# Second MLP: first and second products' matmuls alternate one by one, and the first products' two PSUM banks change places each step

## The chip, the cores and the metric

One core of one Trainium2 chip runs the whole program. The metric is the device time of one execution in microseconds; the median of three executions of the kernel before is 850.15 us (850.1 to 851.2).

## What is computed

The reference runs windowed attention over 4 batches of 8 heads with 576 positions of 64 values, and passes the result, as 2304 tokens of 512 values, through two MLPs with a hidden width of 2048:

```python
def _moe_ref(x, w_in, w_out):            # first MLP
    h = np.maximum(x @ w_in, 0.0)
    return (h * h @ w_out).astype(np.float32)

def _moe2_ref(x, w_in, w_out):           # second MLP
    h = x @ w_in
    g = h * np.cos(h)
    return (g @ w_out).astype(np.float32)
```

## The kernel before

Attention takes the first 100 us or so. Both MLPs work in steps: a block of 768 tokens has 8 steps, each for 256 hidden columns. Step numbers n run from 0 to 47; `FRESH` = 24 is the first of the second MLP, `second(n)` says whether n is in it, and j = n % 8 is the place in the block.

**First products** (x times w_in, `hidden_product(n, i)`, line 706). A 2 by 2 block product is made with seven products, not eight. Each is six matmuls of 384 columns: two halves of the contraction, and for each hi*hi, hi*lo and lo*hi of values split in a rounded and a rest part. Product i writes PSUM bank i % 2. Products 0, 1 and 4 start a fresh sum, the others add on top of what lies in their bank, so each bank has to be read out at the right moment: ScalarE copies the result of product 0 to `part_a` (`copy_part`, line 882, semaphore `part_a_ready`) and that of product 2 to `hidden_sum` (`copy_first_sum`, line 886); VectorE adds in `part_b_sum`, `part_c_sum`, `c22_sum`, `c21_sum` and `c12_sum` (lines 1286 to 1301, in this order `sum_done` goes up by five a step) after products 1, 3, 4, 5, 6. The waits of TensorE stand in lines 723 to 734: product 0 for all five sums of the step before, product 2 for `part_a`, 3 for part_b_sum, 4 for copy_first_sum, 5 for part_c_sum, 6 for c22_sum.

**Between the products.** The hidden values of a step lie in four quarters i of 384 columns. In the second MLP each passes h * cos(h) by nine instructions of the two engines: ScalarE `turns` and `whole` (number of full turns, line 937), VectorE `turn_high` and `turn_low` (take them off, line 1307), ScalarE `absolute` and `cosine` (line 955), VectorE `make_g` (times h, line 1320), ScalarE `round_g` (rounded part, line 965), VectorE `lo_g` (rest part, line 1335). Quarter 0 comes from copy_first_sum, 1 from c22_sum, 2 from c21_sum, 3 from c12_sum.

**Second products** (g times w_out, `second_product(q)`, line 756). Two for each step, each of six pieces of three matmuls with 512 columns in the second MLP. It is a Python generator that gives one piece at a time. `mlp_step(n)` (line 803) runs the seven first products and puts pieces behind them as `pieces_after` says: the six pieces of product 2n-4 (`old`) and then the six of 2n-1 (`new`). Inside the second MLP, but for j = 1 and 2, that is six pieces after product 2 and six after product 6: two rows. `new` needs quarters 1 and 2 of step n-1.

**What sets the order.** Each engine runs its own instruction list, written out by hand; `second_step(n)` has one for ScalarE (line 1027) and one for VectorE (line 1468). Semaphores with constant counts join the lists. SyncE starts all loads in its own order. Beside the quarters, both lists carry `round_moving`, `moving_sum` and `split_moving`, which prepare the next block's operands.

Of the kernel before, what the change touches and what calls it, by code (L numbers as in the profile page):

```python
# [6 lines left out]

# [2 lines left out]

# [6 lines left out]
ALU = mybir.AluOpType  # L19
# [99 lines left out]
def attention_mlp_kernel(nc, q_t, k_t, v, w_in1, w_out1, w_in2, w_out2, out):  # L119
    with ExitStack() as ctx:  # L120
# [170 lines left out]
        def second(n):  # L291

            return n >= ALL // 2

        def slab(q):

# [270 lines left out]
        def _(pe):  # L567
# [135 lines left out]
                last = product(1, 8, keys_at(1, 3 * P + HALF, upper), TAIL_AT[1] + HALF, final=True)  # L703
                last.then_inc(pv_done, 1)

            def hidden_product(n, i):

                t, r = n // STEPS, n % 2
                weight, moving = PRODUCTS[i].split("*")
                w, m = COMB.index(weight), moving  # L710
                if n < MADE:
                    if i < 2:
                        pe.wait_ge(comb_ready, 2 * n + i + 1)
                elif i in GROUP_FIRST:
                    pe.wait_ge(comb_landed[r][GROUP_FIRST[i]], 16 * ((n - MADE) // 2 + 1))
                if n == 0:
                    if m in FIRST_LO_POOL:
                        pe.wait_ge(first_lo_ready, FIRST_LO_POOL[m])
                    if m in FIRST_LO_DVE:
                        pe.wait_ge(xt_ready, FIRST_LO_DVE.index(m) + 1)  # L720
                elif n % STEPS == 0:
                    pe.wait_ge(xt_ready, lo_done(t, m))
                if i == 0 and n > 0:
                    pe.wait_ge(sum_done, 5 * n)
                elif i == 2:
                    pe.wait_ge(part_a_ready, n + 1)
                elif i == 3:
                    pe.wait_ge(sum_done, 5 * n + 1)
                elif i == 4:
                    pe.wait_ge(first_sum_ready, n + 1)  # L730
                elif i == 5:
                    pe.wait_ge(sum_done, 5 * n + 2)
                elif i == 6:
                    pe.wait_ge(sum_done, 5 * n + 3)
                first = i in (0, 1, 4)
                for k in range(2):
                    cols = slice(k * P, k * P + P)
                    hi, lo = comb[:, r, 0, w, cols], comb[:, r, 1, w, cols]
                    for wi, mi in ((hi, moving_hi(t, m)), (hi, moving_lo(t, m)), (lo, moving_hi(t, m))):
                        last = pe.matmul(psum[:, H_BANK + i % 2, 0:NH], wi, mi[:, k, :], start=first, stop=True,  # L740
                                         skip_group_check=True)
                        first = False
                last.then_inc(product_done, 1)

            def wait_for_bank(t, c):

# [9 lines left out]
            def second_product(q):  # L756

                n, r = q // 2, q % W_RING
                t, start = n // STEPS, q % (2 * STEPS) == 1
                final = q == FINAL  # L760
                wo, wl = wout[:, r, 0, :], wout[:, r, 1, :]
                for c in range(6 if second(n) else 4):
                    if c == 0:
                        if second(n):
                            pe.wait_ge(wout_landed[r], 16 * (q // W_RING + 1))
                        else:
                            pe.wait_ge(wout_ready, y_order(q))
                        pe.wait_ge(g_ready, 4 * n + (3 if q % 2 else 4))
                    if start and t > 0:
                        wait_for_bank(t, c)  # L770
                    if second(n):
                        tok = slice(c * P, c * P + P)
                        for m, (g, w) in enumerate(((g_hi, wo), (g_hi, wl), (g_lo, wo))):
                            last = pe.matmul(psum[:, Y_BANK + c, :], g[:, r, tok], w, start=start and m == 0, stop=True,  # L774
                                             skip_group_check=True)
                    else:
                        w = slice(c * P, c * P + P)
                        for m, (wi, g) in enumerate(((wo, g_hi), (wo, g_lo), (wl, g_hi))):
                            pe.matmul(psum[:, Y_BANK + c, :], wi[:, w], g[:, r, 0:512], start=start and m == 0, stop=True,  # L779
                                      skip_group_check=True)  # L780
                            last = pe.matmul(psum[:, Y_BANK + 4 + c // 2, 256 * (c % 2):256 * (c % 2) + 256], wi[:, w],  # L781
                                             g[:, r, 512:N], start=start and m == 0 and c % 2 == 0, stop=True,
                                             skip_group_check=True)
                    if c == (5 if second(n) else 3):
                        last.then_inc(second_done, 1)
                    elif final:
                        last.then_inc(y_done, 1)
                    yield

            def pieces_after(n, i):  # L790

                old, new = second(n - 2), second(n - 1)
                if n <= 2:
                    return ((0, 1, 1, 1, 1, 0, 1), (1, 1, 0, 0, 1, 1, 2))[n - 1][i]
                if n % STEPS == 1:
                    if i < 2:
                        return 3 if old else 2
                    return ((0, 0, 2, 2, 2) if new else (0, 1, 1, 1, 1))[i - 2]
                if old:
                    return ((2, 1, 2, 1, 2, 2, 2) if n % STEPS == 2 else (0, 0, 6, 0, 0, 0, 6))[i]  # L800
                return (1, 1, 1, 1, 1, 1, 2)[i]

            def mlp_step(n):
                old = second_product(2 * n - 4) if n > 2 else zeroth
                new = second_product(2 * n - 1) if n > 1 else first
                olds = 2 if n % STEPS == 1 and n > 1 else 4
                for i in range(len(PRODUCTS)):
                    hidden_product(n, i)
                    for _ in range(pieces_after(n, i)):
                        if n == 1:  # L810
                            next(new if i < 4 else old)
                        else:
                            next(old if i < olds else new)

            zeroth, first = second_product(0), second_product(1)

# [24 lines left out]
            values(PAIRS - 1)  # L841
            hidden_product(0, 6)
            pe.wait_ge(x_ready, PAIRS)
            next(first)
            for n in range(1, ALL):
                mlp_step(n)
            for q in (2 * ALL - 4, 2 * ALL - 1, FINAL):
# [4 lines left out]
        def _(act):  # L852
# [28 lines left out]

            def copy_part(n):
                act.wait_ge(product_done, 7 * n + 1)
                act.activation(part_a[:], psum[:, H_BANK, 0:NH], ACT.Copy).then_inc(part_a_ready, 1)  # L884

            def copy_first_sum(n):

                act.wait_ge(product_done, 7 * n + 3)
                if n > 0:
                    act.wait_ge(g_done, 4 * (n - 1) + 1)  # L890
                act.activation(hidden_sum[:, 0, :], psum[:, H_BANK, 0:NH], ACT.Copy).then_inc(first_sum_ready, 1)

            def weights_hi(n):
                r = n % 2
# [132 lines left out]
            def second_step(n):  # L1027
                t, j = divmod(n, STEPS)
                if n == FRESH:
                    copy_part(n)  # L1030
                    round_g(n - 1, 2)
                    round_wout(2 * n - 2)
                    round_g(n - 1, 3)
                else:
                    whole(n - 1, 3)
                    if n < ALL:
                        copy_part(n)
                    round_g(n - 1, 1)
                    absolute(n - 1, 2)
                    cosine(n - 1, 2)  # L1040
                    round_g(n - 1, 2)
# [70 lines left out]
        def _(dve):  # L1112
# [166 lines left out]
                dve.tensor_tensor(wout[:, r, 1, :], wout_raw[:, r, 1, :], wout[:, r, 0, :].bitcast(F32), ALU.subtract)\  # L1279
                    .then_inc(wout_ready, 1)  # L1280

            def sum_of(n, product, bank, left, to):
                dve.wait_ge(product_done, 7 * n + product + 1)
                dve.tensor_tensor(to, psum[:, H_BANK + bank, 0:NH], left, ALU.add).then_inc(sum_done, 1)  # L1284

            def part_b_sum(n):
                dve.wait_ge(part_a_ready, n + 1)
                sum_of(n, 1, 1, part_a[:], part_b[:])

            def part_c_sum(n):  # L1290
                sum_of(n, 3, 1, part_a[:], part_c[:])

            def c22_sum(n):
                dve.wait_ge(sum_done, 5 * n + 2)
                sum_of(n, 4, 0, part_c[:], hidden_sum[:, 1, :])

            def c21_sum(n):
                sum_of(n, 5, 1, part_a[:], hidden_sum[:, 2, :])

            def c12_sum(n):  # L1300
                sum_of(n, 6, 0, part_b[:], hidden_sum[:, 3, :])

            def quarter(n, i):

# [163 lines left out]
            def second_step(n):  # L1468
                t, j = divmod(n, STEPS)
                if n == FRESH:  # L1470
# [2 lines left out]
                    split_wout(2 * n - 2)  # L1473
                    lo_g(n - 1, 3)
                    split_at(n)
                else:
                    make_g(n - 1, 1)
                    turn_low(n - 1, 2)
                    lo_g(n - 1, 1)
                    turn_high(n - 1, 3)  # L1480
# [97 lines left out]
```

## Time and profile before

| | us |
|---|---|
| median of three executions | 850.15 |
| the profiled execution | 850.42 |
| its span | 848.3 |
| TensorE busy in the span | 836.8 |
| VectorE busy | 647.5 |
| ScalarE busy | 520.3 |
| one step (step 39) | 15.60 |

The span is from the first to the last instruction of the profiled execution. A busy share is an average over all stages; the second MLP runs from about 458 us to the end. Step 39 starts at 691.9 us.

### The profile page before, as it was taken

To read this page: it belongs to the slowest core of one execution; us is meant where nothing else is said; L and a number is where in the kernel's file an instruction comes from. 1 tells how busy PE (TensorE), PEld (TensorE's weight loads), DVE (VectorE), ACT (ScalarE), POOL (GpSimd) and SP (SyncE) were. 2 spreads that over 40 slices of the span, in tenths; PEclk is the share of its full clock that TensorE was granted. 3 is DMA by queue.
4 is the path that set the end of the run, shared out by engine and by line. 5 is a ranking of instruction groups with operands and counts; after the bars stand their busy time and mean duration, and the time that the engine had idled before them with its cause. 6 is when DMAs were issued, how large, how long until landed. Compare 5 with 4: busy or idle time off the path is not lost.

```text
span 848.3 us, 16158 instructions
## 1 busy us (share of the span) xinstructions
PE 836.8 (99%) x5846; PEld 759.9 (90%) x5846; DVE 647.5 (76%) x1448; ACT 520.3 (61%) x1148; POOL 84.4 (10%) x177
## 2 busy tenths in 40 slices
PE   8999999999999999999999999999999999999998
PEld 6777999999999999999999999899889989899996
DVE  7999888886696775786766787777787677677665
ACT  7999454432343333344333887877787777787775
POOL 7999400000000000000000000000000000000000
PEclk9999999999999999999999999999999999999999
DMA  7776736457679779769868556555575655675522
GB/s 245 253 255 183 254 117 245 173 170 276 226 271 321 254 244 322 275 238 317 288 242 295 182 198 200 182 171 194 189 254 181 200 183 175 211 241 177 191 75 75
DMA packets 72190, 185.34 MB, mean 218 GB/s; under 512 B 7216, under 2 KB 19760, under 8 KB 70064
## 3 DMA queue, kind: packets, MB, share of 16 engines
q1 hardware_dynamic: 71248, 183.23, 64.2%
q10 hardware_dynamic: 864, 1.08, 0.4%
q8 instruction: 47, 0.77, 0.4%
q14 instruction: 31, 0.25, 0.1%
HBM read 141.82 MB, written 42.47 MB: 217 GB/s over the span
## 4 chain that ended last, share of the span: by engine, by line
PE 89%; DVE 7%; POOL 2%; issue 1%; ACT 1%; DVEq 0%; POOLq 0%
PE psum L740 40%; PE psum L774 23%; PE psum L779 15%; PE psum L781 8%; DVE probs L1152 3%; POOL probs L528 2%; DVE pt L1172 1%; DVE guarded L1161 1%; PE psum L632 1%; PE psum L679 1%; PE psum L574 1%; DVE x L1180 0%; ACT probs L861 0%; DVE x L1179 0%; PE psum L591 0%
## 5 line engine op out<-in xcount | busy, mean ns | idle before, releaser
L740 PE MATMUL psum<-xt_hi,comb 128*128 128x384 f32 x1344 | 381.3, 336 | 0.2
L740 PEld LDWEIGHTS psum<-xt_hi,comb 128*128 128x128 f32 x1344 | 246.4, 188 | 10.7 <-DVE hidden_sum L1284 0.4
L774 PE MATMUL psum<-wout,g_hi 128*128 128x512 f32 x576 | 178.4, 391 | 0.0
L1338 DVE TENSOR_TENSOR g_lo<-work,g_hi 128x384 fp32r<-128x384 f32 x192 | 102.4, 552 | 74.1 <-ACT g_hi L971 72.7
L779 PE MATMUL psum<-g_hi,wout 128*128 128x512 f32 x384 | 148.8, 391 | 0.0
L971 ACT ACTIVATE g_hi<-work 128x384 fp32r<-128x384 f32 x192 | 97.6, 519 | 70.1 <-DVE work L1333 42.2
L740 PE MATMUL psum<-x_lo,comb 128*128 128x384 f32 x384 | 128.6, 335 | 0.0
L774 PEld LDWEIGHTS psum<-wout,g_hi 128*128 128x128 f32 x576 | 107.2, 188 | 19.0
L774 PE MATMUL psum<-wout,g_lo 128*128 128x512 f32 x288 | 113.2, 393 | 0.0
L781 PE MATMUL psum<-g_hi,wout 128*128 128x256 f32 x384 | 107.5, 280 | 0.0
L884 ACT ACTIVATE part_a<-psum 128x384 f32<-128x384 f32 x48 | 23.6, 491 | 125.5 <-PE psum L740 125.5
L740 PE MATMUL psum<-xt_lo,comb 128*128 128x384 f32 x288 | 96.6, 335 | 0.0
L779 PEld LDWEIGHTS psum<-g_hi,wout 128*128 128x128 f32 x384 | 71.9, 187 | 9.0
L779 PE MATMUL psum<-g_lo,wout 128*128 128x512 f32 x192 | 75.1, 391 | 0.0
L740 PEld LDWEIGHTS psum<-x_lo,comb 128*128 128x128 f32 x384 | 72.2, 188 | 1.6
L947 ACT ACTIVATE angle<-hidden_sum,consts 128x384 f32<-128x384 f32 x96 | 58.4, 609 | 22.8 <-DVE hidden_sum L1284 21.9
L781 PEld LDWEIGHTS psum<-g_hi,wout 128*128 128x128 f32 x384 | 72.4, 188 | 0.0
L528 POOL TENSOR_SCALAR probs<-probs,inverse 128x128 f32<-128x128 f32 (+1 forms) x144 | 68.7, 498 | 9.6 <-DVE inverse L1164 9.6
L861 ACT ACTIVATE probs<-probs,neg_max 128x128 f32<-128x128 f32 (+1 forms) x144 | 61.9, 438 | 4.2 <-DVE neg_max L1152 4.2
L774 PEld LDWEIGHTS psum<-wout,g_lo 128*128 128x128 f32 x288 | 54.0, 188 | 11.4
L1311 DVE SCALAR_TENSOR_TENSOR work<-angle,hidden_sum 128x384 f32<-128x384 f32 x96 | 52.9, 551 | 13.9 <-ACT angle L953 13.9
L1284 DVE TENSOR_TENSOR part_b<-psum,part_a 128x384 f32<-128x384 f32 x48 | 26.6, 554 | 48.3 <-PE psum L740 48.3
(99 smaller groups left out, 1267.6 us busy)
## 6 DMA issues: line engine op xcount, KB each, us to landing
comb<-comb SPq DMA_DIRECT2D x80, 768.0 KB, 5.6
wout<-wout SPq DMA_DIRECT2D x48, 512.0 KB, 3.3
comb<-comb SPq DMA_DIRECT2D x8, 1792.0 KB, 6.8
comb<-kept SPq DMA_DIRECT2D x8, 1792.0 KB, 6.9
wout_raw<-w_out SPq DMA_DIRECT2D x48, 256.0 KB, 5.7
comb<-comb SPq DMA_DIRECT2D x40, 256.0 KB, 3.2
v_raw<-v SPq DMA_DIRECT2D x16, 512.0 KB, 3.5
raw<-w_in SPq DMA_DIRECT2D x32, 256.0 KB, 7.2
```

The source lines that it names most:

```text
L528: pool.tensor_scalar(m, m, inverse[:, r, u:u + 1], 1.0, ALU.mult, ALU.mult).then_inc(probs_ready, 1)
L740: last = pe.matmul(psum[:, H_BANK + i % 2, 0:NH], wi, mi[:, k, :], start=first, stop=True, skip_group_check=True)
L774: last = pe.matmul(psum[:, Y_BANK + c, :], g[:, r, tok], w, start=start and m == 0, stop=True, skip_group_check=True)
L779: pe.matmul(psum[:, Y_BANK + c, :], wi[:, w], g[:, r, 0:512], start=start and m == 0, stop=True, skip_group_check=True)
L781: last = pe.matmul(psum[:, Y_BANK + 4 + c // 2, 256 * (c % 2):256 * (c % 2) + 256], wi[:, w], g[:, r, 512:N], start=start and m == 0 and c ...
L861: act.activation(m, m, ACT.Exp, bias=neg_max[:, r, u:u + 1], scale=-1.0, accum_out=row_sum[:, r, u:u + 1]).then_inc(exp_ready, 1)
L947: act.activation(angles[i][:], hidden_sum[:, i, :], ACT.Identity, bias=consts[:, 1:2], scale=1.0 / (2.0 * math.pi)).then_inc(turns_ready, 1)
L971: act.activation(g_hi[:, r, cols], work[i][:], ACT.Copy).then_inc(g_hi_ready, 1)
L1152: dve.tensor_tensor_reduce(probs_of(p, u), score_of(u), at, -SCALE, 3e38, ALU.add, ALU.min, neg_max[:, r, u:u + 1]).then_inc(biased, 1)
L1284: dve.tensor_tensor(to, psum[:, H_BANK + bank, 0:NH], left, ALU.add).then_inc(sum_done, 1)
L1311: dve.scalar_tensor_tensor(out=work[i][:], in0=angles[i][:], scalar=-TURN_HI, in1=hidden_sum[:, i, :], op0=ALU.mult, op1=ALU.add).then_inc ...
L1338: dve.tensor_tensor(g_lo[:, r, cols], work[i][:], g_hi[:, r, cols].bitcast(F32), ALU.subtract)\
```

## The change

Four edits go together.
- In 16 steps of the second MLP, those for which `mixed(n)` holds (27 to 32, 35 to 40, 43 to 46), each of the first five matmuls of a first product is followed by one second matmul, and in product 6 also the sixth. The order among the first matmuls, and among the second, stays. `second_product` now gives one matmul at a time (in the first MLP a 512 and 256 pair), and `one_piece` takes three.
- Product i of step n writes bank (n + i) % 2 in all steps of both MLPs, not i % 2. With seven products a step the banks then take turns without a break.
- Product 0 waits for four of the five sums of the step before, product 1 for the fifth.
- ScalarE's and VectorE's lists have a new order in mixed steps, and the steps after one begin with the instructions that it left over (`turns` 3; `c12_sum`, `turn_high` 2).

```diff
+        def mixed(n):
+
+            return second(n - 2) and n < ALL - 1 and n % STEPS not in (1, 2)
+
+        def hidden_bank(n, i):
+
+            return H_BANK + (n + i) % 2
...
-                if i == 0 and n > 0:
-                    pe.wait_ge(sum_done, 5 * n)
+                if i < 2 and n > 0:
+                    pe.wait_ge(sum_done, 5 * n - 1 + i)
...
-                        last = pe.matmul(psum[:, H_BANK + i % 2, 0:NH], wi, mi[:, k, :], start=first, stop=True,
+                        last = pe.matmul(psum[:, hidden_bank(n, i), 0:NH], wi, mi[:, k, :], start=first, stop=True,
                                          skip_group_check=True)
                         first = False
-                last.then_inc(product_done, 1)
+                        if k == 1 and wi is lo:
+                            last.then_inc(product_done, 1)
+                        yield
...
+                pieces = itertools.chain(new, old) if n == 1 else itertools.chain(old, new)
                 for i in range(len(PRODUCTS)):
...
+                    if mixed(n):
+                        for k, _ in enumerate(hidden_matmuls(n, i)):
+                            if k < 5 or i == 6:
+                                next(pieces)
+                    else:
+                        hidden_product(n, i)
+                        one_piece(pieces, pieces_after(n, i))
...
+                elif mixed(n):          # ScalarE
+                    round_g(n - 1, 1)
+                    if mixed(n - 1):
+                        turns(n - 1, 3)
+                    absolute(n - 1, 2)
+                    cosine(n - 1, 2)
+                    copy_part(n)
+                    whole(n - 1, 3)
+                    round_g(n - 1, 2)
+                    absolute(n - 1, 3)
+                    cosine(n - 1, 3)
+                    round_g(n - 1, 3)
+                    copy_first_sum(n)
+                    turns(n, 0)
+                    whole(n, 0)
+                    if t + 1 < 2 * SUPERS:
+                        for name in HI_AT[j]:
+                            round_moving(t + 1, name)
+                    absolute(n, 0)
+                    cosine(n, 0)
+                    round_g(n, 0)
+                    turns(n, 1)
+                    whole(n, 1)
+                    turns(n, 2)
+                    absolute(n, 1)
+                    cosine(n, 1)
+                    whole(n, 2)
+                    return
                 else:
+                    if mixed(n - 1):
+                        turns(n - 1, 3)
                     whole(n - 1, 3)
...
+                elif mixed(n):          # VectorE
+                    make_g(n - 1, 1)
+                    if mixed(n - 1):
+                        c12_sum(n - 1)
+                        turn_high(n - 1, 2)
+                    turn_low(n - 1, 2)
+                    lo_g(n - 1, 1)
+                    make_g(n - 1, 2)
+                    turn_high(n - 1, 3)
+                    turn_low(n - 1, 3)
+                    part_b_sum(n)
+                    lo_g(n - 1, 2)
+                    make_g(n - 1, 3)
+                    if T_AT[j] and t + 1 < 2 * SUPERS:
+                        moving_sum(t + 1, T_AT[j])
+                    lo_g(n - 1, 3)
+                    split_at(n)
+                    turn_high(n, 0)
+                    part_c_sum(n)
+                    turn_low(n, 0)
+                    make_g(n, 0)
+                    c22_sum(n)
+                    lo_g(n, 0)
+                    turn_high(n, 1)
+                    c21_sum(n)
+                    turn_low(n, 1)
+                    return
                 else:
                     make_g(n - 1, 1)
+                    if mixed(n - 1):
+                        c12_sum(n - 1)
+                        turn_high(n - 1, 2)
                     turn_low(n - 1, 2)
```

## Rows read from the trace of the kernel before

**Rows 1.** The page: busy time and share of each engine; clock in 40 slices.

```profile
PE 836.8 (99%) x5846; PEld 759.9 (90%) x5846; DVE 647.5 (76%) x1448; ACT 520.3 (61%) x1148; POOL 84.4 (10%) x177
PEclk9999999999999999999999999999999999999999
```

**Rows 2.** Busy time by stretch: attention, a first-MLP step, steps 27 to 46, step 39.

```profile
core 0: us, PE busy (x) PEld busy (x) DVE busy (x) ACT busy (x) POOL busy (x), PEclk, DMA share, GB/s
8.00:20.00 12.00, 9.66 (x182) 7.64 (x184) 10.10 (x68) 12.00 (x53) 8.17 (x21) 1.00 0.95 316
442.00:457.60 15.60, 15.60 (x92) 14.61 (x91) 10.84 (x19) 5.07 (x9) 0.00 (x0) 1.00 0.83 301
504.50:816.90 312.40, 312.40 (x1562) 282.21 (x1560) 230.55 (x448) 241.50 (x462) 0.00 (x0) 1.00 0.60 192
691.90:707.50 15.60, 15.60 (x79) 14.11 (x78) 11.31 (x23) 11.61 (x23) 0.00 (x0) 1.00 0.62 194
```

**Rows 3.** The chain of waits from 690 us: start, length, line, matmuls.

```profile
695.21 4.12 PE psum L774 x18
699.33 4.21 PE psum L740 x24
...
707.66 3.14 PE psum L740 x18
```

**Rows 4.** Timeline of VectorE in step 39: start, length, line, operands.

```profile
694.58 0.55 DVE L1311 SCALAR_TENSOR_TENSOR work<-angle,hidden_sum 128x384 f32<-128x384 f32 x1
695.05 0.55 DVE L1284 TENSOR_TENSOR part_b<-psum,part_a 128x384 f32<-128x384 f32 x1
695.51 0.55 DVE L1325 TENSOR_TENSOR work<-hidden_sum,angle 128x384 f32<-128x384 f32 x1
...
698.33 0.56 DVE L1311 SCALAR_TENSOR_TENSOR work<-angle,hidden_sum 128x384 f32<-128x384 f32 x1 [0.46 <-ACT angle L953]
698.92 0.56 DVE L1317 SCALAR_TENSOR_TENSOR angle<-angle,work 128x384 f32<-128x384 f32 x1
...
701.54 0.56 DVE L1284 TENSOR_TENSOR hidden_sum<-psum,part_c 128x384 f32<-128x384 f32 x1 [0.55 <-PE psum L740]
...
706.73 0.56 DVE L1325 TENSOR_TENSOR work<-hidden_sum,angle 128x384 f32<-128x384 f32 x1 [0.31 <-ACT angle L963]
```

**Rows 5.** Timeline of ScalarE in step 39.

```profile
693.16 0.49 ACT L884 ACTIVATE part_a<-psum 128x384 f32<-128x384 f32 x1 [0.90 <-PE psum L740]
693.55 0.52 ACT L971 ACTIVATE g_hi<-work 128x384 fp32r<-128x384 f32 x1
693.97 0.52 ACT L958 ACTIVATE angle<-angle 128x384 f32<-128x384 f32 x1
694.51 0.62 ACT L963 ACTIVATE angle<-angle,consts 128x384 f32<-128x384 f32 x1
696.09 0.53 ACT L971 ACTIVATE g_hi<-work 128x384 fp32r<-128x384 f32 x1 [0.96 <-DVE work L1325]
696.52 0.47 ACT L891 ACTIVATE hidden_sum<-psum 128x384 f32<-128x384 f32 x1
697.03 0.62 ACT L947 ACTIVATE angle<-hidden_sum,consts 128x384 f32<-128x384 f32 x1
697.68 0.62 ACT L953 ACTIVATE angle<-angle,consts 128x384 f32<-128x384 f32 x1
...
699.51 0.53 ACT L958 ACTIVATE angle<-angle 128x384 f32<-128x384 f32 x1
700.07 0.62 ACT L963 ACTIVATE angle<-angle,consts 128x384 f32<-128x384 f32 x1
...
702.13 0.62 ACT L947 ACTIVATE angle<-hidden_sum,consts 128x384 f32<-128x384 f32 x1 [1.45 <-DVE hidden_sum L1284]
...
706.09 0.62 ACT L963 ACTIVATE angle<-angle,consts 128x384 f32<-128x384 f32 x1
706.61 0.60 ACT L947 ACTIVATE angle<-hidden_sum,consts 128x384 f32<-128x384 f32 x1
```

**Rows 6.** The page's costliest groups: busy us, mean ns, idle before.

```profile
L740 PEld LDWEIGHTS psum<-xt_hi,comb 128*128 128x128 f32 x1344 | 246.4, 188 | 10.7 <-DVE hidden_sum L1284 0.4
```

More of the change, by code:

```diff
@@ L10 @@
+import itertools
 import math
@@ L704, in values, with hidden_matmuls @@
                 last.then_inc(pv_done, 1)
-            def hidden_product(n, i):
+            def hidden_matmuls(n, i):
                 t, r = n // STEPS, n % 2
@@ L739, in hidden_product @@
                     for wi, mi in ((hi, moving_hi(t, m)), (hi, moving_lo(t, m)), (lo, moving_hi(t, m))):
-                        last = pe.matmul(psum[:, H_BANK + i % 2, 0:NH], wi, mi[:, k, :], start=first, stop=True,
+                        last = pe.matmul(psum[:, hidden_bank(n, i), 0:NH], wi, mi[:, k, :], start=first, stop=True,
                                          skip_group_check=True)
                         first = False
-                last.then_inc(product_done, 1)
+                        if k == 1 and wi is lo:
+                            last.then_inc(product_done, 1)
+                        yield
+            def hidden_product(n, i):
+                for _ in hidden_matmuls(n, i):
+                    pass
             def wait_for_bank(t, c):
@@ L775, in second_product @@
                                              skip_group_check=True)
+                            if m < 2:
+                                yield
                     else:
@@ L783, in second_product @@
                                              skip_group_check=True)
+                            if m < 2:
+                                yield
                     if c == (5 if second(n) else 3):
@@ L805, in mlp_step, with one_piece @@
                 new = second_product(2 * n - 1) if n > 1 else first
-                olds = 2 if n % STEPS == 1 and n > 1 else 4
+                pieces = itertools.chain(new, old) if n == 1 else itertools.chain(old, new)
                 for i in range(len(PRODUCTS)):
[L808 to L813, printed above, removed]
+                    if mixed(n):
[5 more added lines that the diff above has]
+                        one_piece(pieces, pieces_after(n, i))
+            def one_piece(pieces, count=1):
+                for _ in range(3 * count):
+                    next(pieces)
             zeroth, first = second_product(0), second_product(1)
@@ L843, in _ @@
             pe.wait_ge(x_ready, PAIRS)
-            next(first)
+            one_piece(first)
             for n in range(1, ALL):
@@ L883, in copy_part @@
                 act.wait_ge(product_done, 7 * n + 1)
-                act.activation(part_a[:], psum[:, H_BANK, 0:NH], ACT.Copy).then_inc(part_a_ready, 1)
+                act.activation(part_a[:], psum[:, hidden_bank(n, 0), 0:NH], ACT.Copy).then_inc(part_a_ready, 1)
             def copy_first_sum(n):
@@ L890, in copy_first_sum @@
                     act.wait_ge(g_done, 4 * (n - 1) + 1)
-                act.activation(hidden_sum[:, 0, :], psum[:, H_BANK, 0:NH], ACT.Copy).then_inc(first_sum_ready, 1)
+                act.activation(hidden_sum[:, 0, :], psum[:, hidden_bank(n, 2), 0:NH], ACT.Copy).then_inc(first_sum_ready, 1)
             def weights_hi(n):
@@ L1280, in split_wout, with sum_of @@
                     .then_inc(wout_ready, 1)
-            def sum_of(n, product, bank, left, to):
+            def sum_of(n, product, left, to):
                 dve.wait_ge(product_done, 7 * n + product + 1)
-                dve.tensor_tensor(to, psum[:, H_BANK + bank, 0:NH], left, ALU.add).then_inc(sum_done, 1)
+                dve.tensor_tensor(to, psum[:, hidden_bank(n, product), 0:NH], left, ALU.add).then_inc(sum_done, 1)
             def part_b_sum(n):
                 dve.wait_ge(part_a_ready, n + 1)
-                sum_of(n, 1, 1, part_a[:], part_b[:])
+                sum_of(n, 1, part_a[:], part_b[:])
             def part_c_sum(n):
-                sum_of(n, 3, 1, part_a[:], part_c[:])
+                sum_of(n, 3, part_a[:], part_c[:])
             def c22_sum(n):
                 dve.wait_ge(sum_done, 5 * n + 2)
-                sum_of(n, 4, 0, part_c[:], hidden_sum[:, 1, :])
+                sum_of(n, 4, part_c[:], hidden_sum[:, 1, :])
             def c21_sum(n):
-                sum_of(n, 5, 1, part_a[:], hidden_sum[:, 2, :])
+                sum_of(n, 5, part_a[:], hidden_sum[:, 2, :])
             def c12_sum(n):
-                sum_of(n, 6, 0, part_b[:], hidden_sum[:, 3, :])
+                sum_of(n, 6, part_b[:], hidden_sum[:, 3, :])
             def quarter(n, i):
```

## The prediction

> **What bounds the kernel now.** I began with the busy shares [rows 1]: TensorE is busy 99% of the span at a granted clock of nine tenths or more in every slice, ahead of VectorE (76%) and ScalarE (61%). The change touches the second MLP alone, so I then read that stage in stretches [rows 2]. From 504.5 to 816.9 us (steps 27 to 46) TensorE is busy 312.4 of 312.4 us, at clock 1.00; VectorE has 230.6 (74%) and ScalarE 241.5 (77%). One step, such as 39, takes 15.60 us. The reader should note the two second shares: with a quarter of the time free, both can still become the bound if their work is ordered so that they wait for each other.
>
> The chain of waits in that stage runs over TensorE only [rows 3]: 18 first matmuls in 3.14 us, 18 second in 4.12, 24 first in 4.21, 18 second in 4.12. That is 0.175 us a first matmul (384 columns), 0.229 a second (512). Six first matmuls are thus 1.05 us, a piece (three second matmuls) 0.69. The rows after these repeat it.
>
> Last I read the timelines of VectorE and ScalarE through step 39 for one thing, the time from the start of one instruction to the start of the next, as it depends on what joins them [rows 4, 5]:
> - VectorE, the next needs nothing: 0.47 (694.58, 695.05, 695.51). The next needs the result: 0.59 (698.33, 698.92).
> - VectorE to ScalarE: 0.59 (698.92 to 699.51; 701.54 to 702.13), after make_g 0.58 (695.51 to 696.09).
> - ScalarE to VectorE: whole to turn_high 0.65 (697.68 to 698.33), cosine to make_g 0.64 (706.09 to 706.73).
> - ScalarE, next needs the result: turns to whole 0.65, absolute to cosine 0.54 and 0.56, so 0.55. Needs nothing: 0.52 after one of 0.62 us (706.09, 706.61), 0.39 after copy_part, 0.43 round_g to copy_first_sum, and 0.51 from there to turns, which needs it.
>
> **The change part by part.**
>
> *Order of the matmuls.* Steps 27 to 32, 35 to 40 and 43 to 46 are mixed: 16. Nothing is added or dropped: 42 first and 36 second matmuls, 42 × 0.175 + 36 × 0.229 = 15.6. Product i now comes due every 6 × 0.175 + 5 × 0.229 = 2.195 us, the last at 13.17 us after the step's start.
>
> *Banks and waits.* Product 0 no longer waits for the last sum of the step before; product 1 does. In steps without mixing nothing is idle there today [rows 2], so this gives nothing. The price of a wait that is late is what it is late by, plus 0.03 and a weight load of 0.188 us [rows 6]: I take 0.22.
>
> *Order on ScalarE and VectorE.* This is the part that decides. Both queues run in the order written, so I laid the two new orders of a steady mixed step side by side and followed the latest predecessor of each instruction. TensorE's products turn out never to be it. What is left is a closed chain that changes engine 12 times. With starts in us after that of make_g(n-1, 1), by the times above:
> V: c12_sum 0.47, turn_high 2 0.94, turn_low 2 1.53. S: absolute 2 2.12, cosine 2 2.67, copy_part(n) 3.19, whole 3 3.58. V: turn_high 3 4.23, turn_low 3 4.82. S: absolute 3 5.41, cosine 3 5.96. V: make_g 3 6.60. S: round_g 3 7.18, copy_first_sum(n) 7.61, turns 0 8.12, whole 0 8.77. V: turn_high 0 9.42, part_c_sum 9.89, turn_low 0 10.36. S: absolute 0 10.95, cosine 0 11.50. V: make_g 0 12.14, c22_sum 12.61. S: turns 1 13.20, whole 1 13.85. V: turn_high 1 14.50, c21_sum 14.97. S: turns 2 15.56, absolute 1 16.08, cosine 1 16.63. V: make_g(n, 1) 17.27.
>
> That start opens the next step's chain, so a mixed step can't be shorter than 17.27 us, against 15.60 of TensorE's work: 1.67 us lost. TensorE stands before the products that wait for the chain: product 1 (c12_sum of the step before), 2 (copy_part), 5 (part_c_sum) and 6 (c22_sum). Round_moving, moving_sum and split_moving (0.8 to 1 us) lie in gaps where an engine waits for the other, so I price them at nothing; where a gap is too short each costs at most its own length in one step.
>
> Why has today's order no such chain? There turn 3 of step n-1, quarter 0 of step n and the sums are interwoven, so that two quarters are under way at once and the round trips overlap. The new order finishes nearly one quarter before the next begins.
>
> *The ends of each run of mixed steps.* In 27, 35 and 43 the chain is entered late enough: product 0 ends at 5 × (0.175 + 0.229) + 0.33 = 2.35, copy_part starts at 2.38, make_g(n, 1) 17.27 - 3.19 = 14.08 later, at 16.46. That is 0.86 into the next step (28, 36, 44). There c22_sum ends at 0.86 + 12.61 + 0.56 = 14.03 and product 6 starts at 14.25, not 13.17: 1.1 lost. From then on all 1.67: steps 29 to 32, 37 to 40, 45 and 46, ten of them. After each run a step in the old order inherits the lag. In a bound step product 6 starts at 12.61 + 0.56 + 0.22 = 13.39, the step ends 6 × (0.175 + 0.229) = 2.42 later, at 15.81, so make_g(46, 1) starts 1.46 into step 47. Its c12_sum ends at 2.49, product 1 starts at 2.71 where it was due at 1.05 (1.66), and product 2 waits for copy_part behind turns 3 and whole 3, 0.63 more: 2.3. In steps 33 and 41 product 1 comes after three pieces and is not late; product 4 is, by copy_first_sum behind two copies of finished output: 1.3 and 0.4 by the same walk (step 33 has also moving work for a next block, step 41 none).
>
> Sum: 10 × 1.67 + 3 × 1.1 + 2.3 + 1.3 + 0.4 = 24.0 us.
>
> *The pace of matmuls one by one.* Rows 2 and 3 show no 384 alternating with a 512. Nearest is the first MLP, where a 512 and a 256 alternate: its step [rows 2] has 90 matmuls over the same 34,560 columns, also 15.60 us. At 2.4 GHz (clock 1.00) the columns are 14.4 us, so it pays 13.3 ns a matmul, and the second MLP's 78 pay 15.4. Alternation at 13.3 gives 15.44, -0.16 a step; the other bound is nothing on top of the columns, -1.2. Dearer changes of shape, say +0.25 a step, are the upper one. While the chain sets 17.27, TensorE has 1.67 us to spare and neither end counts, but for steps 27, 35 and 43 (-0.5 to +0.8 in all). I take nothing.
>
> The Trainium skill (TensorE: Matmul & The Clock Gate, "Wait — 56ns, not 53.3ns?") gives a warm matmul its columns plus about 2.5 ns, with which a mixed step would be 14.6 us, an estimate from that page. The rows pay 13 to 15 ns, so they don't bear it out, and the sum would be the same by either, as the chain hides it.
>
> The profiled execution took 850.42 us with a span of 848.3; the median is 850.15. Forecast: 850.15 + 24.0, **874.1 us**.
>
> **Rivals.**
> *A, faster.* The chain doesn't bind: it would have to be under 15.44 us, 11% less, by quicker hand-overs. Then only the even pace remains: 16 × -0.16 = -2.6, 847.6 us; with nothing on top of columns 16 × -1.2 = -19, 831. Against it: each hand-over is read from a row of this very code. 6%.
> *B, no change.* A chain between 15.5 and 15.65 us and pace unchanged: 850. 3%.
> *C, part of it.* I have one hand-over in four too dear, or the real order slips past one engine change. A round trip to the other engine is 0.59 + 0.64 = 1.2 us. With 16.6 us a step it is 10 × 1.0 + 3 × 0.5 + 2.5 = 14, 864 us. 5%.
> *D, transfers.* The second products of step n-2 now end at 7.9 us of a step and not 7.3, so the loads of output weights behind them start later, and SP's queue with them. They are wanted a whole step later, so there are 8 us of room for 3.3 to 5.6. If it fails, a wait of some 2 us in a dozen steps: 890 and over. 1%.
> *E, the clock falls.* The new order brings TensorE four short stands a step. Today's clock is 1.00 even from 8 to 20 us, with TensorE busy 9.66 of 12 us [rows 2], more idle than the 10% I forecast. At 1.2 GHz a step would be twice 15.6 us, +14 × 16 = over 1,090 us. 1%. The Trainium skill (same page, "A second HAM failure mode: psum-queue depth-cycling") says that cycling through PSUM banks with small idles between matmul groups makes the clock swing; by that rule E would be the outcome, and no row here does so.
>
> **How the numbers follow.** The forecast has 84%. Its own range is 869 to 878: 0.02 us on a third of the 31 hand-overs is 0.2 a step, 2.6 in all, and the ends of the runs may be off by 2. Taking in most of C, the range is 863 to 880. A kernel like this can't be told from no change within 0.2% (1.7 us). Faster is A, 6%; same is B, 3%; slower is the rest, 91%.
>
> **What would show it.** Right: in 504 to 820 us TensorE is no longer fully busy, with idle before products 1, 2, 5 and 6 put down to VectorE's sums and ScalarE's part_a; steps of 17.2 to 17.3 us inside a run and 15.6 in steps 34, 42; the chain of waits passes through VectorE and ScalarE; no wait of theirs on TensorE's products in steps 29 to 32. Wrong: mixed steps at 15.4 to 15.6 (A, B), idle put down to DMA (D), a granted clock under 1 (E), or VectorE and ScalarE idle before sums on a late product, which would mean a loop through TensorE that I haven't seen.

## The result, and the profile after

The changed kernel takes 874.76 us (median of five executions, 874.14 to 875.02), the kernel before 850.56 in the same comparison: ratio 1.0282, 95% interval 1.0271 to 1.0294. It is slower by 24.2 us, where 24.0 were forecast (874.1 us). Its profiled execution has a span of 872.9 us, 24.6 more than before.

The page shows the same instructions, and TensorE a little less busy [rows 1]:

```profile
PE 852.6 (98%) x5846; PEld 756.1 (87%) x5846; DVE 652.7 (75%) x1448; ACT 525.0 (60%) x1148; POOL 84.1 (10%) x177
PEclk9999999999999999999999999999999999999999
```

Share of busy time says nearly nothing here: 99% became 98%. One reason is that a matmul's record is 0.33 us long where the next may start after 0.17, so that a short stand of the engine vanishes in it. The stretches show it by their length. These are step 27, step 39, the whole of 27 to 46, and step 47 to the end. Before, step 39 took 15.60 us and steps 27 to 46 took 312.4 [rows 2]:

```profile
504.76:520.68 15.92, 15.92 (x80) 14.19 (x78) 11.62 (x21) 11.61 (x22) 0.00 (x0) 1.00 0.53 178
705.91:723.21 17.30, 16.75 (x79) 13.75 (x79) 11.68 (x23) 11.81 (x23) 0.00 (x0) 1.00 0.50 167
504.76:839.21 334.45, 327.44 (x1561) 277.90 (x1560) 233.78 (x444) 243.57 (x457) 0.00 (x0) 1.00 0.53 180
839.21:872.90 33.69, 28.57 (x133) 23.97 (x132) 18.75 (x38) 20.11 (x39) 0.00 (x0) 1.00 0.23 78
```

Step 39 begins with the first matmul of product 0 at 705.91 us and ends with that of step 40 at 723.21: 17.30 us.

The chain of waits through that stretch no longer holds a matmul [rows 3]. Columns are start, time on the chain, engine, tile, line; here from make_g of step 38's quarter 1 (L1379) to that of step 39's quarter 0, without the pieces of up to 0.03 us between them:

```profile
707.42 0.04 DVE work L1379
707.45 0.44 issue
707.89 0.55 DVE hidden_sum L1338
708.44 0.48 DVE work L1365
708.94 0.57 DVE angle L1371
709.53 0.53 ACT angle L982
710.12 0.50 issue
710.62 0.47 ACT part_a L908
711.09 0.51 ACT angle L977
711.62 0.57 DVE work L1365
712.22 0.57 DVE angle L1371
712.81 0.54 ACT angle L982
713.37 0.62 ACT angle L987
714.02 0.57 DVE work L1379
...
715.04 0.48 ACT hidden_sum L915
715.55 0.63 ACT angle L971
716.20 0.62 ACT angle L977
716.85 0.56 DVE work L1365
717.40 0.47 DVE part_c L1338
717.87 0.48 DVE angle L1371
718.37 0.53 ACT angle L982
718.93 0.63 ACT angle L987
719.58 0.03 DVE work L1379
```

The reader should see two engines handing over to each other the whole way, and the same order as in the prediction. The lines say "issue" where the next instruction on its own engine merely follows. The chain closes: make_g of step 39's quarter 1 starts at 724.72, 17.30 us after that of step 38.

```profile
724.72 0.56 DVE L1379 TENSOR_TENSOR work<-hidden_sum,angle 128x384 f32<-128x384 f32 x1 [1.28 <-ACT angle L987]
```

What TensorE's weight loads stand and wait for in step 39 (in brackets: idle, releaser):

```profile
708.50 0.19 PEld L749 LDWEIGHTS psum<-xt_hi,comb 128*128 128x128 f32 x1 [0.57 <-DVE hidden_sum L1338]
711.14 0.19 PEld L749 LDWEIGHTS psum<-xt_hi,comb 128*128 128x128 f32 x1 [0.54 <-ACT part_a L908]
717.99 0.19 PEld L749 LDWEIGHTS psum<-xt_hi,comb 128*128 128x128 f32 x1 [0.26 <-issue]
720.66 0.19 PEld L749 LDWEIGHTS psum<-xt_hi,comb 128*128 128x128 f32 x1 [0.57 <-DVE hidden_sum L1338]
```

These are products 1, 2, 5 and 6. For product 5 the profile names no releaser, but part_c_sum had ended 0.12 us before (717.32 and 0.55), and TensorE loses only some 0.1 us there. The waits of 504 to 823 us, in total, times and longest, are led by the two engines waiting for each other, not for TensorE, and none is for a DMA:

```profile
DVE work L1379 <- ACT angle L987: 53.7, 61, 1.3
ACT angle L982 <- DVE angle L1371: 38.5, 49, 1.6
...
PEld psum L749 <- DVE hidden_sum L1338: 9.6, 17, 0.6
```

Where the 24.6 us lie, by the starts of product 0 in the two traces:

| steps | us a step after (before) | more |
|---|---|---|
| 27, 35, 43 | 15.91 (15.57) | 1.0 |
| 28, 36, 44 | 16.5 (15.62) | 2.6 |
| 29 to 32, 37 to 40, 45, 46 | 17.25 to 17.39 (15.60 to 15.63) | 17.0 |
| 33, 41 | 16.79, 15.95 (15.69) | 1.4 |
| 34, 42 | 15.69 (15.69) | 0 |
| 47 to the end | 33.7 (31.4) | 2.3 |

The remaining 0.25 us lie ahead of step 27.

### The profile page after: what moved, and what is told of

It is laid out like the page before. It is cut to its first block, busy times and chain, and to the rows that moved or that the text cites. A ratio compares the mean times of both kernels' runs of the same rounds, so it can differ in the third digit from the quotient of the medians.

```text
span 872.9 us, 16170 instructions
## 1 busy us (share of the span) xinstructions
PE 852.6 (98%) x5846; PEld 756.1 (87%) x5846; DVE 652.7 (75%) x1448; ACT 525.0 (60%) x1148; POOL 84.1 (10%) x177
## 4 chain that ended last, share of the span: by engine, by line
PE 59%; DVE 18%; ACT 15%; issue 5%; POOL 2%; DVEq 0%; POOLq 0%; ACTq 0%
PE psum L749 26%; PE psum L796 15%; PE psum L789 8%; PE psum L798 8%; DVE work L1365 4%; ACT angle L971 3%; ACT angle L982 3%; ACT angle L987 3%; DVE hidden_sum L1338 3%; ACT angle L977 3%; DVE probs L1206 3%; DVE angle L1371 3%; POOL probs L537 2%; DVE work L1379 1%; ACT hidden_sum L915 1%
## 5 line engine op out<-in xcount | busy, mean ns | idle before, releaser
L749 PE MATMUL psum<-xt_hi,comb 128*128 128x384 f32 x1344 | 409.3, 340 | 9.0 <-DVE hidden_sum L1338 6.0
L749 PEld LDWEIGHTS psum<-xt_hi,comb 128*128 128x128 f32 x1344 | 248.9, 188 | 39.9 <-DVE hidden_sum L1338 12.8
L789 PE MATMUL psum<-wout,g_hi 128*128 128x512 f32 x576 | 211.7, 394 | 0.0
L1379 DVE TENSOR_TENSOR work<-hidden_sum,angle 128x384 f32<-128x384 f32 x96 | 53.4, 557 | 61.5 <-ACT angle L987 61.1
L982 ACT ACTIVATE angle<-angle 128x384 f32<-128x384 f32 x96 | 49.9, 520 | 43.7 <-DVE angle L1371 43.7
```

The lines of the kernel that those rows point to most:

```text
L749: last = pe.matmul(psum[:, hidden_bank(n, i), 0:NH], wi, mi[:, k, :], start=first, stop=True, skip_group_check=True)
L982: act.activation(a, a, ACT.Abs).then_inc(abs_ready, 1)
L1379: dve.tensor_tensor(w, h, angles[i][:], ALU.mult).then_inc(g_done, 1)
```

## Experiments

The theory is the chain: with the new lists of ScalarE and VectorE a step takes at least 17.3 us, however early TensorE's products come. Its rivals are that the order of the matmuls makes the loss (evenly spaced products whose results are fetched late), or the banks and waits.

**Banks and waits alone.** `mixed` is false for every step.

```diff
-            return second(n - 2) and n < ALL - 1 and n % STEPS not in (1, 2)
+            return False
```

> The banks changing places and the split wait of products 0 and 1, in every step, with no mixed step: rows of matmuls and the lists of ScalarE and VectorE as before. Chain theory: the lists decide, so nothing moves, 849.8 to 850.9 us, steps of 15.60. Rival (banks): the new bank order or the later wait of product 1 costs part of the 24 us; then over 852 us here.

Measured 850.07 us against 850.49, ratio 0.9996 (0.9986 to 1.0005). With the old rows and lists the banks and the split wait neither cost nor give.

**Matmuls alone, lists as before.** ScalarE's and VectorE's `mixed(n)` are replaced by a function that is always false.

```diff
-                elif mixed(n):
+                elif relisted(n):     # ScalarE and VectorE; always False
```

> Banks and the one-by-one order of matmuls as in the change, but ScalarE and VectorE keep their lists of before. Chain theory: the chain of 17.2 to 17.3 us is gone, TensorE is the bound again at the pace seen in step 27 of the changed kernel, 15.91 us, so 16 x 0.31 = 5 us and up to 2.5 us at the ends of the runs, where the old lists are a little late: 855 to 858.5 us. Rival (matmul order): evenly spaced products make each eviction late, whatever the lists; then 870 us or more.

Measured 857.01 us, ratio 1.0074 (1.0054 to 1.0095). Steps inside a run take 15.92 us, the first and the last of one up to 16.17. The one-by-one order is thus worth 6.5 us of loss by itself, and the other 17.7 of the 24.2 come with the lists.

**Lists alone, matmuls in two rows.**

```diff
-                    if mixed(n):
+                    if False:         # TensorE only
```

> Banks and the new lists of ScalarE and VectorE, but the matmuls in two rows as before. Chain theory: the chain stays and now also has TensorE's rows in it, because products 3 to 6 come only after the first row of second matmuls and the second row needs quarters 1 and 2: steps of 17.4 to 18.2 us, 880 to 887 us. Rival (matmul order): without the alternation the loss is gone or mostly gone, 850 to 856 us.

Measured 884.87 us, ratio 1.0402 (1.0381 to 1.0423); steps of 17.65 to 18.0 us. The lists lose more with the old rows than with the order that they were written for: the two parts of the change are no sum (6.5 and 34.4 against 24.2). Here TensorE's rows have become links of the loop. The chain of waits goes from copy_part through product 2, the row of 18 second matmuls and product 3 to part_c_sum, where the changed kernel's goes from copy_part on over VectorE and ScalarE:

```profile
559.96 0.48 ACT part_a L908
...
560.48 1.33 PE psum L749 x6
561.80 4.12 PE psum L789 x18
565.92 1.08 PE psum L749 x6
...
567.03 0.56 DVE part_c L1338
```

**One pair exchanged.** In mixed steps VectorE runs c12_sum first.

```diff
                 elif mixed(n):
-                    make_g(n - 1, 1)
                     if mixed(n - 1):
                         c12_sum(n - 1)
+                    make_g(n - 1, 1)
+                    if mixed(n - 1):
                         turn_high(n - 1, 2)
```

> The changed kernel with one pair of VectorE's instructions exchanged in mixed steps: c12_sum of the step before ahead of make_g of quarter 1. It takes 0.42 us net out of the chain (TensorE's product 1 and turns of quarter 3 are released before make_g). Chain theory: steps in a run 16.85 to 16.9 us where they were 17.30, the second step of a run 16.1 where it was 16.5; in all 5 to 6 us less than the changed kernel, 869 to 870 us. Rival (matmul order or a TensorE loop): one exchanged pair of 0.47 us moves nothing, 874 to 875 us.

Measured 869.17 us, ratio 1.0217 (1.0197 to 1.0238). The row of step 39, 16.87 us long where it was 17.30:

```profile
702.62:719.49 16.87, 16.49 (x80) 13.81 (x79) 11.72 (x23) 11.75 (x23) 0.00 (x0) 1.00 0.52 171
```

One place in one list moves the kernel 5.6 us. The matmul-order rival can't explain that.

**A term of the chain made shorter.** `absolute` works on half its columns and leaves the other half as it was, so the output differs.

```diff
+                if mixed(n) and (mixed(n + 1) or i < 2):
+                    a = angles[i][:, 0:NH // 2]
                 act.activation(a, a, ACT.Abs).then_inc(abs_ready, 1)
```

> The changed kernel, but `absolute` works on 192 of the 384 columns in mixed steps (the other half is left as it was, so the output differs). Four `absolute` are in the chain of a step, each about 0.17 us shorter by the rows of ScalarE's copies of 256 and 512 columns (370 and 595 ns). Chain theory: every term counts one to one, 4 x 0.17 = 0.68 less a step, 16.6 us in place of 17.30, 864 to 866 us in all. Rival (TensorE's order or its waits set the step): no change, 874 to 875 us.

Measured 865.54 us, ratio 1.0178 (1.0157 to 1.0198). One such instruction takes 361 ns, against 520 at full width in the changed kernel; four times 0.159 is 0.64, and the steps fell from 17.30 to 16.66, by 0.64:

```profile
L984 ACT ACTIVATE angle<-angle 128x192 f32<-128x192 f32 x16 | 5.8, 361 | 9.7 <-DVE angle L1373 9.7
```

**Four pairs exchanged.** Beside the first: turn_low 0 ahead of part_c_sum and c21_sum ahead of turn_high 1 on VectorE, copy_first_sum ahead of round_g 3 on ScalarE.

```diff
-                    round_g(n - 1, 3)
                     copy_first_sum(n)
+                    round_g(n - 1, 3)
...
-                    part_c_sum(n)
                     turn_low(n, 0)
+                    part_c_sum(n)
...
-                    turn_high(n, 1)
                     c21_sum(n)
+                    turn_high(n, 1)
```

> The changed kernel with four pairs exchanged in mixed steps: c12_sum ahead of make_g 1, turn_low 0 ahead of part_c_sum, c21_sum ahead of turn_high 1 on VectorE, copy_first_sum ahead of round_g 3 on ScalarE. By the times between starts, the longest chain falls from 17.27 to under 15.9 us, so TensorE is the bound at its own pace for one-by-one matmuls, 15.91 to 15.95 us a mixed step: 16 x 0.32 = 5.1, and 1.3 to 2.2 at steps 33 and 47, 857 to 858 us. Rival (the lists can't be mended so lightly, or TensorE's order has a share of the 17.30): steps over 16.3, 863 us or more.

Measured 856.62 us, ratio 1.0074 (1.0058 to 1.0091), just under the range expected. The chain is off the path, with no instruction removed; a step is 15.92 us, with TensorE busy throughout:

```profile
552.00:567.92 15.92, 15.92 (x80) 14.19 (x79) 11.90 (x23) 12.55 (x24) 0.00 (x0) 1.00 0.53 182
```

Since this and the old lists both end at 15.92, that is what one-by-one matmuls cost TensorE. It is dearer than the 15.60 of two rows. The remaining four runs ask why.

**Two by two, and three by three**, with the old lists:

```diff
-                            if k < 5 or i == 6:
-                                next(pieces)
+                            if i > 0 and k % 2 == 1:        # threes: k % 3 == 2
+                                for _ in range(2):          # threes: 3
+                                    next(pieces)
```

> The lists of before with matmuls taking turns two by two (two first, two second) behind products 1 to 6 of mixed steps; product 0 is not interleaved, with which no wait is late. What is asked is the pace alone. Switch theory: each change from a second matmul to a first costs one 13.3 ns slot, which one by one is 36 a step (0.48 us over 15.44); two by two it is 18, 15.68 us a step, 851.5 to 852.5 us with 0.7 for the last step. Rival (a fixed dearer second matmul, 237 ns wherever a first one is near): 15.9, 855 to 856 us.

> As the kernel with pairs, but three first and three second matmuls take turns, behind products 1 to 6. Two by two cost 13.3 ns for each first and second matmul, as one by one did; rows of six cost 32 ns for twelve. If the extra slot is for every 896 columns of mixed work, whatever the grain, threes take 15.9 us a step and 856 us again; if it is for each change of kind, threes lie between, at 15.75 to 15.8 us, 853.5 to 854.5 us.

Pairs: 855.96 us, ratio 1.0065 (1.0045 to 1.0085), steps of 15.92. The theory of a slot for each switch is wrong there: half the switches, the same price. The time is that of the rival, a dearer second matmul wherever a first one is near (here 235 ns in the mean). Threes: 852.48 us, ratio 1.0027 (1.0015 to 1.0039), steps of 15.72, which neither theory gave; there the second matmuls take 232 ns in the mean. The price falls with coarser rows, but not as their number.

**Second matmuls narrowed to 384 columns**, one by one with the old lists, to make the widths equal. A quarter of the second products' output is left out:

```diff
+                            width = NH if mixed(n + (1 if q % 2 else 2)) else DM
-                            last = pe.matmul(psum[:, Y_BANK + c, :], g[:, r, tok], w, ...
+                            last = pe.matmul(psum[:, Y_BANK + c, 0:width], g[:, r, tok], w[:, 0:width], ...
```

> Matmuls one by one with the lists of before, but the second matmuls of mixed steps stream 384 of 512 columns (a quarter of their output is left out), so that both kinds are equally wide. Width theory of the pace (the extra slot comes from two widths taking turns): a pair takes 2 x 173.3 = 346.7 ns. Alternation theory (it comes from the two kinds taking turns, whatever their width): 360 ns, one slot of 13.3 more, as 413.3 against 400 in the kernel with 512. Steps are then no measure, since ScalarE and VectorE come near to being the bound (14.5 us); the gaps between matmuls are.

The first fence is TensorE one by one with 384 and 512 columns (old lists), the second with 384 and 384; first column start.

```profile
543.99 0.40 PE L793 MATMUL psum<-wout,g_hi 128*128 128x512 f32 x1
544.23 0.34 PE L753 MATMUL psum<-xt_hi,comb 128*128 128x384 f32 x1
544.41 0.40 PE L793 MATMUL psum<-wout,g_lo 128*128 128x512 f32 x1
544.64 0.34 PE L753 MATMUL psum<-xt_hi,comb 128*128 128x384 f32 x1
544.82 0.40 PE L793 MATMUL psum<-wout,g_hi 128*128 128x512 f32 x1
```

```profile
542.16 0.33 PE L794 MATMUL psum<-wout,g_hi 128*128 128x384 f32 x1
542.33 0.33 PE L753 MATMUL psum<-xt_hi,comb 128*128 128x384 f32 x1
542.51 0.33 PE L794 MATMUL psum<-wout,g_hi 128*128 128x384 f32 x1
542.68 0.33 PE L753 MATMUL psum<-xt_hi,comb 128*128 128x384 f32 x1
542.85 0.33 PE L794 MATMUL psum<-wout,g_lo 128*128 128x384 f32 x1
```

Two pairs take 0.83 us above, two take 0.69 below: 346 ns a pair, so no slot is added. The two kinds may take turns for nothing if their widths are equal. (The whole kernel took 831.17 us in one execution; with a quarter of the columns gone, that says nothing of the pace.)

**First matmuls narrowed to 256 columns**, so that 256 and 512 take turns. A third of each first product is left out:

```diff
+                        width = 256 if mixed(n) else NH
-                        last = pe.matmul(psum[:, hidden_bank(n, i), 0:NH], wi, mi[:, k, :], ...
+                        last = pe.matmul(psum[:, hidden_bank(n, i), 0:width], wi, mi[:, k, 0:width], ...
```

> Matmuls one by one with the lists of before, but the first matmuls of mixed steps stream 256 of their 384 columns (a third of each first product is left out), so the widths that take turns are 256 and 512. Any-two-widths theory: whenever widths differ, a pair of a first and a second matmul costs one slot of 13.3 ns more than 120.0 + 226.7 = 346.7 ns, so 360. Particular-widths theory: as 256 and 512 take turns for nothing in the first MLP, where the two also share their weights, a pair takes 346.7 here too and the extra slot belongs to 384 with 512. Only the gaps between matmuls are asked; the step is then bound by ScalarE and VectorE, at some 14.5 us or less.

```profile
547.10 0.39 PE L794 MATMUL psum<-wout,g_hi 128*128 128x512 f32 x1
547.33 0.28 PE L754 MATMUL psum<-x_lo,comb 128*128 128x256 f32 x1
547.44 0.39 PE L794 MATMUL psum<-wout,g_hi 128*128 128x512 f32 x1
547.67 0.28 PE L754 MATMUL psum<-xt_hi,comb 128*128 128x256 f32 x1
547.79 0.39 PE L794 MATMUL psum<-wout,g_lo 128*128 128x512 f32 x1
```

Two pairs are 0.69 us, 345 ns each. Unequal widths as such are not the cause either: of the three pairs of widths tried, only 384 with 512 pays the slot. Both free pairs have 768 columns and this one has 896, so the runs don't tell whether it goes by the two widths or by their sum. Why, no run shows. (This kernel took 830.57 us in one execution, with work left out.) No kernel here that does all the work is faster than the one before.

## Why the prediction was right

*The chain.* Its 31 terms, each from a row of before, gave 17.27 us; the step takes 17.30. Term by term too: counted from make_g at 707.42, copy_part was put at 3.19 and starts at 3.20, make_g 3 at 6.60 and 6.60, copy_first_sum 7.61 and 7.62, turn_high 0 at 9.42 and 9.43, make_g 0 at 12.14 and 12.16. That it is the cause is shown from three sides: the matmul order alone costs 6.5 us and the banks nothing, while the other 17.7 come only with the lists; one pair exchanged moves a step by 0.43 us; four terms shortened by 0.64 together shorten it by 0.64.

*Which products stand waiting.* Products 1, 2, 5 and 6, as forecast, though 5 for only some 0.1 us. The price of a late wait was put at 0.22 us; product 1 starts 0.06 after the end of c12_sum, and its next first matmul comes 0.51 later where 0.41 is the pace: about 0.16.

*Work said to be covered.* Round_moving, moving_sum and split_moving were priced at nothing. Step 39 has a split_moving (0.95 us at 715.64) and still takes 17.30, equal to the other bound steps to within 0.1 us.

*The ends of the runs.* Steps 28, 36 and 44 together lose 2.6 us where 3.3 was said, the two steps 33 and 41 1.4 for 1.7, the end 2.3 for 2.3.

*The pace of the matmuls.* The one term that was mis-sized. Nothing was taken, the dear bound was +0.25 us a step; measured is +0.32 in a step that TensorE bounds (15.92 against 15.60), outside that bound. I had called the first MLP's 512 and 256 the nearest row and so expected alternation to be cheap; the run with 256 columns shows that this pair is a free one and 384 with 512 is not. It hardly shows in the sum, since ten of the sixteen mixed steps are set by the chain: 1.0 us in steps 27, 35 and 43. In the sum its +1.0 and the -1.0 at the ends of the runs offset each other. By the chain's own logic two thirds of that are not luck, though no run tests it alone: the chain is entered in the first step of a run, so what step 27 takes longer is less to lose in 28, and the two together took 32.4 us where 32.3 were forecast. The 0.3 at steps 33 and 41 is luck, against 0.3 that the ten bound steps lose more than said (17.0 for 16.7).

*The rivals.* A counted on 847.6 us if the chain didn't bind. With four pairs exchanged it doesn't, and the kernel takes 856.6: that rival had the wrong pace.

*The Trainium skill's rules.* The Trainium skill (TensorE: Matmul & The Clock Gate, "Wait — 56ns, not 53.3ns?") gives a warm matmul its columns plus about 2.5 ns. The rows here don't agree: a settled matmul pays 13.3 ns over its columns, and the alternating pairs of 384 and 512 more. The Trainium skill (same page, "A second HAM failure mode: psum-queue depth-cycling") tells of a kernel whose clock swings as it cycles through PSUM banks with small idles between groups of matmuls. Here it did not: the granted clock was 1.00 in step 39, with four stands in 17.30 us.

## What to carry to other kernels

Where two helper engines pass data back and forth, their busy shares (74% and 77% in steps 27 to 46 before the change) don't tell whether they can keep up. Write one period of both lists side by side, follow the latest predecessor of each instruction until the chain closes on itself, and add up the times from start to start; that is a floor for the step, to be compared with the bottleneck's own time, and exchanging two independent neighbours on the chain can be a cheap cure: one pair took 0.43 us off a step here, and four took the chain off the path. When an interleaving is meant to even out an engine's load, measure the pace of the interleaved instructions by itself as well: here it was a loss even with good lists.

## What the runs showed of the hardware that was not expected

- TensorE, 384- and 512-column matmuls taking turns one by one or two by two: 413 ns a pair (15.92 us a step is 0.48 over 15.44, by 36 pairs 13.3 ns each), where settled rows of one kind in the kernel before have 173.3 and 226.7 ns (400); threes are between (15.72 us a step). With 384 and 384 a pair is 346 ns, with 256 and 512 345: 768 columns at 2.4 GHz are 320 ns, and twice 13.3 makes 346.7, nothing added. The cause of the slot is open.
- The first matmuls after a change of kind are dearer even in long rows. In step 39 before the change the nine first 512s after a row of 384s take some 40 ns more together, the six first 384s after a row of 512s some 26. With two rows of each kind that is 0.13 us of the 0.16 by which the step's 15.60 us exceeds 42 × 173.3 + 36 × 226.7 ns = 15.44. The other 0.03 lies further on in the row of 24 first matmuls.
